# mLSTM-style attention with two MLP layers, 1 core: probabilities times v as one plain fp32 product per head

## What is computed

```
for t in range(S):                                   # the reference, a recurrence per (batch, head)
    C = f_stab * C + i_stab * outer(v_t, k_t)        # 40 x 40 state
    n = f_stab * n + i_stab * k_t
    y_t = sigmoid(o_gate_t) * (C q_t) / max(|n q_t|, 1)
x = prelu(x @ w_in, alpha) @ w_out                   # layer 1: 320 -> 2048 -> 320
out = max(x @ w1, x @ w2, x @ w3) @ w_out2           # layer 2: 320 -> 768 (three times) -> 320
```

## Time and profile before

| | us |
|---|---|
| median of 3 runs (lowest, highest) | 805.46 (802.93, 806.68) |
| span of the profiled execution, first to last instruction | 803.0 |
| PE busy in it | 754.5 (94%) |
| DVE busy | 541.9 (67%) |
| ACT busy | 298.8 (37%) |
| POOL busy | 206.7 (26%) |
| one pass of the loop (of 7) | 59.44 |

### The profile page before, as it was taken

The page is one execution under the profiler, slowest core; times in us unless marked ns, Lnnn a source line. Parts: engine busy times, 40 slices in busy tenths (PEclk is TensorE's granted clock), DMA queues, the critical chain, the costliest instruction groups (busy, mean ns, idle before and its releaser), DMA issues.

```text
span 803.0 us, 13943 instructions
## 1 busy us (share of the span) xinstructions
PE 754.5 (94%) x4658; PEld 702.0 (87%) x4658; DVE 541.9 (67%) x870; ACT 298.8 (37%) x685; POOL 206.7 (26%) x206
## 2 busy tenths in 40 slices
PE   1659999999999999999999999699999999999997
PEld 1649999999999999999999998698888888888886
DVE  7697997997997997997988985934243342434222
ACT  3535436436436436436435435331211212121211
POOL 5382432432433333333333312700000000000000
PEclk9968999999999999999999999999999999999999
DMA  6970321321311212222210009011020202000000
GB/s 197 279 236 18 119 69 41 118 67 46 113 67 62 97 67 82 77 67 89 70 67 24 0 0 283 6 39 65 1 72 1 72 0 72 0 33 1 33 1 33
DMA packets 37145, 55.93 MB, mean 70 GB/s; under 512 B 3329, under 2 KB 27458, under 8 KB 36738
## 3 DMA queue, kind: packets, MB, share of 16 engines
q1 hardware_dynamic: 36690, 54.57, 21.1%
q10 hardware_dynamic: 432, 1.06, 0.5%
HBM read 47.65 MB, written 7.96 MB: 69 GB/s over the span
## 4 chain that ended last, share of the span: by engine, by line
PE 70%; DVE 20%; issue 5%; DMA 1%; ACT 1%; SPq 1%; DVEq 0%; POOL 0%; ACTq 0%
PE bank L640 25%; PE bank L597 16%; DVE scale L936 4%; PE bank L613 4%; DVE g_lo L953 4%; PE bank L615 4%; PE bank L614 3%; PE bank L533 3%; PE bank L653 3%; PE bank L654 3%; PE bank L655 3%; DVE g_full L965 2%; PE bank L618 2%; PE bank L617 2%; DVE inner L910 2%
## 5 line engine op out<-in xcount | busy, mean ns | idle before, releaser
L597 PE MATMUL bank<-x_split,w_hi 128*128 128x384 f32 x640 | 182.9, 351 | 0.7 <-ACT x_split L738 0.7
L597 PE MATMUL bank<-x_split,w_lo 128*128 128x384 f32 x384 | 130.7, 340 | 0.0
L597 PEld LDWEIGHTS bank<-x_split,w_hi 128*128 128x128 f32 x640 | 119.1, 191 | 2.9 <-DVE g_full L965 1.8
L953 DVE TENSOR_TENSOR g_lo<-g_full,g_hi 128x384 fp32r<-128x384 f32 x128 | 104.7, 818 | 23.1 <-ACT g_hi L773 22.1
L773 ACT ACTIVATE g_hi<-g_full 128x384 fp32r<-128x384 f32 x128 | 66.6, 520 | 133.9 <-DVE g_full L965 133.9
L613 PE MATMUL bank<-g_hi,wproj 128*128 128x384 f32 x256 | 94.7, 370 | 8.9 <-DVE g_lo L953 8.1
L757 ACT ACTIVATE g_full<-bank 128x384 f32<-128x384 f32 x128 | 62.5, 488 | 99.2 <-PE bank L597 99.1
L1002 DVE TENSOR_TENSOR best<-bank,first_of_max 128x512 f32<-128x512 f32 x36 | 24.9, 692 | 108.1 <-PE bank L640 81.3
L965 DVE SCALAR_TENSOR_TENSOR g_full<-g_full,beta,bank 128x384 f32<-128x384 f32 x128 | 77.8, 608 | 17.5 <-ACT g_full L757 17.5
L615 PE MATMUL bank<-g_hi,wproj 128*128 128x384 f32 x256 | 87.0, 340 | 0.0
L614 PE MATMUL bank<-g_lo,wproj 128*128 128x384 f32 x256 | 86.7, 339 | 0.0
(11 more groups left out here) (115 smaller groups left out, 1506.1 us busy)
## 6 DMA issues: line engine op xcount, KB each, us to landing
u_bcast<-u_scratch SPq DMA_DIRECT2D x24, 512.0 KB, 4.3
kvo<-in_kvo SPq DMA_DIRECT2D x24, 484.0 KB, 3.5
out<-final SPq DMA_DIRECT2D x6, 640.0 KB, 3.4
layer_scratch<-rows SPq DMA_DIRECT2D x8, 384.0 KB, 2.4
q_t<-in_q_t SPq DMA_DIRECT2D x24, 120.0 KB
k_t<-in_k_t SPq DMA_DIRECT2D x48, 60.0 KB
wproj_raw<-in_w_out SPq DMA_DIRECT2D x1, 2560.0 KB, 16.7
w_raw<-in_w_max SPq DMA_DIRECT2D x2, 1152.0 KB, 9.7
```

Source lines behind the costliest of these rows:

```text
L597: ins = pe.matmul(ps[:, 0:T], w[:, a, f], xs[:, x, :], start=(m == 0), stop=(m == 7))
L953: dve.tensor_tensor(gl[:, j % G_SLOTS, :], gf[:, j % GF_SLOTS, :], gh[:, j % G_SLOTS, :].bitcast(F32), ALU.subtract).then_inc(g_lo_done, 1)
```

## The change

All values steps now take the form that block 0 had, with 41 columns in the place of 128, and all that served the bf16 parts is gone: the pack steps, prob_rest, prob_3, v_parts, v_rest, their semaphores and memsets, line 926 and the sum at line 910.

```diff
-DVE_LINKS = CPB * (1 + 4 + 3)
+DVE_LINKS = CPB * (1 + 3 + 3)
...
-    att = [[("gate", 0, 0)], [("gate", 0, 1), ("prepare", 1)], [("pack", 0, 0), ("pack", 0, 1)]]
+    att = [[("gate", 0, 0)], [("gate", 0, 1), ("prepare", 1)]]
...
-                [("finish", c, 1)] + more * [("pack", c + 1, 0)],
-                [("finish", c, 2)] + more * [("pack", c + 1, 1)] + later * [("prepare", c + 2)]]
+                [("finish", c, 1)],
+                [("finish", c, 2)] + later * [("prepare", c + 2)]]
...
                 if kind == "values":
-                    if isinstance(blk, int):
-                        pe.wait_ge(nat_loaded[c], 16 * (blk + 1))
-                        pe.wait_ge(prob_done, NG * ch + step[2] + 1)
-                        for k in range(HG):
-                            h = step[2] * HG + k
-                            v = VO + h * DE
-                            ins = pe.matmul(ps[:, k * COLS:(k + 1) * COLS], prob[:, h, :], nat[:, c, v:v + COLS],
-                                            start=True, stop=True)
-                    else:
...
-                            pe.matmul(ps[:, o:o + 3 * DE], high(prob[:, h, :]), v, start=(k == 0), stop=False,
...
-                            pe.matmul(ps[:, o:o + 2 * DE], high(prob_r[:, h, :]), v[:, 0:2 * DE], start=False,
...
-                            ins = pe.matmul(ps[:, o:o + DE], prob_3[:, h, :], v[:, 0:DE], start=False,
...
+                    pe.wait_ge(nat_loaded[c], 16 * (blk + 1))
+                    pe.wait_ge(prob_done, NG * ch + step[2] + 1)
+                    for k in range(HG):
+                        h = step[2] * HG + k
+                        v = VO + h * DE
+                        ins = pe.matmul(ps[:, k * COLS:k * COLS + DE], prob[:, h, :], nat[:, c, v:v + DE],
+                                        start=True, stop=True)
...
-                if kind == "pack":
...
-                        act.activation(v_parts[:, :, 0, 0:D], v, ACT.Copy).then_inc(v_hi, 1)
...
-                        act.activation(v_parts[:, :, 1, 0:D], v_r[:, :, :], ACT.Copy).then_inc(v_mid, 1)
...
-                    if not isinstance(blk, int):
-                        dve.wait_ge(prob_done, NG * ch + g + 1)
-                        dve.tensor_tensor(prob_r[:, heads, :], prob[:, heads, :], high(prob[:, heads, :]), ALU.subtract
-                                          ).then_inc(prob_rest, 1)
...
-                        dve.tensor_reduce(inner[:, heads, :],
-                                          ps[:, 0:HG * 3 * DE].rearrange("p (k n d) -> p k d n", k=HG, n=3),
-                                          mybir.AxisListType.X, ALU.add).then_inc(inner_in, 1)
+                    dve.tensor_tensor(inner[:, heads, :],
+                                      ps[:, :].rearrange("p (k d) -> p k d", k=HG)[:, :, 0:DE],
+                                      before_chunk[:, heads, :], ALU.add).then_inc(inner_in, 1)
...
-                    if not isinstance(blk, int):
-                        link(dve.tensor_tensor(inner[:, :, :], inner[:, :, :], before_chunk[:, 0:H, :], ALU.add))
...
-            pool.memset(v_parts[:, :, :, :], 0.0)
             link(pool.memset(kt[:, 1:CPB, :, :], 0.0))
-            pool.memset(v_parts[:, :, 0, D:DE], 1.0)
...
-                        pool.tensor_tensor(v_r[:, :, :], v, v_parts[:, :, 0, 0:D], ALU.subtract).then_inc(v_rest, 1)
...
-                        pool.tensor_tensor(v_parts[:, :, 2, 0:D], v_r[:, :, :], v_parts[:, :, 1, 0:D], ALU.subtract
...
-                    pool.tensor_tensor(prob_3[:, heads, :], prob_r[:, heads, :], high(prob_r[:, heads, :]), ALU.subtract
```

More of the change, by code:

```diff
@@ L108, in first_plan @@
     for s in PLAN_ATT:
-        if s[0] not in ("prepare", "pack") and not (s[0] == "finish" and s[1] + 1 < CPB):
+        if s[0] != "prepare" and not (s[0] == "finish" and s[1] + 1 < CPB):
             steps.append(s)
@@ L146, in wait @@
         eng.wait_ge(sem, value)
-def high(ap):
-    return ap.bitcast(BF16)[(slice(None),) * (len(ap.shape) - 1) + (slice(1, None, 2),)]
 def of_heads(ps):
@@ L206, in build @@
         prob, _ = sb("prob", [128, H, L], F32)
[L207 to L210, removed]
         v_w, _ = sb("v_weighted", [128, CPB, WG], F32)
@@ L289, in build @@
         decayed = sem("state_decayed")
[L291 to L296, removed]
         gated = sem("gated")
@@ L519, in attention @@
                 kind, c = step[0], step[1]
-                if kind in ("prepare", "gate", "pack", "finish"):
+                if kind in ("prepare", "gate", "finish"):
                     return
@@ L551, in attention @@
                 if kind == "values":
-                    if isinstance(blk, int):
-                        pe.wait_ge(nat_loaded[c], 16 * (blk + 1))
-                        pe.wait_ge(prob_done, NG * ch + step[2] + 1)
-                        for k in range(HG):
-                            h = step[2] * HG + k
-                            v = VO + h * DE
-                            ins = pe.matmul(ps[:, k * COLS:(k + 1) * COLS], prob[:, h, :], nat[:, c, v:v + COLS],
-                                            start=True, stop=True)
-                    else:
[L562 to L566, removed]
-                            pe.matmul(ps[:, o:o + 3 * DE], high(prob[:, h, :]), v, start=(k == 0), stop=False,
-                                      skip_group_check=True)
-                            pe.matmul(ps[:, o:o + 2 * DE], high(prob_r[:, h, :]), v[:, 0:2 * DE], start=False,
-                                      stop=False, skip_group_check=True)
-                            ins = pe.matmul(ps[:, o:o + DE], prob_3[:, h, :], v[:, 0:DE], start=False,
-                                            stop=True, skip_group_check=True)
+                    pe.wait_ge(nat_loaded[c], 16 * (blk + 1))
[5 more added lines that the diff above has]
+                                        start=True, stop=True)
                     ins.then_inc(values_out, 1)
@@ L723, in attention @@
                                    scale=-1.0).then_inc(eo_done, 1)
-                if kind == "pack":
[L726 to L729, removed]
-                        act.activation(v_parts[:, :, 0, 0:D], v, ACT.Copy).then_inc(v_hi, 1)
-                    else:
-                        act.wait_ge(v_rest, ch - CPB + 1)
-                        act.activation(v_parts[:, :, 1, 0:D], v_r[:, :, :], ACT.Copy).then_inc(v_mid, 1)
                 if kind == "turn":
@@ L875, in attention @@
                 ch = blk * CPB + c
-                if kind in ("prepare", "gate", "pack"):
+                if kind in ("prepare", "gate"):
                     return
@@ L1093, in attention @@
                         mask(c, ch)
[L1094 to L1098, removed]
-                        pool.tensor_tensor(v_r[:, :, :], v, v_parts[:, :, 0, 0:D], ALU.subtract).then_inc(v_rest, 1)
-                    else:
-                        pool.wait_ge(v_mid, ch - CPB + 1)
-                        pool.tensor_tensor(v_parts[:, :, 2, 0:D], v_r[:, :, :], v_parts[:, :, 1, 0:D], ALU.subtract
[L1103 to L1107, removed]
-                    pool.tensor_tensor(prob_3[:, heads, :], prob_r[:, heads, :], high(prob_r[:, heads, :]), ALU.subtract
-                                       ).then_inc(prob_split, 1)
                 if kind == "carry":
```

## The result

The changed kernel takes 817.75 us (median of 4 runs, 816.91 to 818.99) against 804.48 for the kernel before: ratio 1.0163, 95% interval [1.0142, 1.0184], or +13.3 us. Measured twice more, on other occasions, it gave 1.0172 [1.0155, 1.0189] and 1.0176 [1.0163, 1.0189]. The forecast was 816.3 in a range of 808 to 822, slower with a chance of 0.81. It holds, though the loss is 2.5 to 3 us larger than the 10.8 I had summed. The profiled execution took 816.91 us, its span 815.1, 12.1 more than the span before. (In each run of the changed kernel the span is 1.7 to 1.8 us shorter than the time, so the 803.0 of before stands for a time of some 804.8, near the middle of its runs and not at their lower end.)

A forecast was written before the change was run, and what follows sets the result against it. The prediction took TensorE's instruction issue to bound layer 1's loop. Dearer values steps, +13.4 us, less 2.6 us of end-of-pass waits gave +10.8 us, on a median of 805.46 us 816.3 us, range 808 to 822.

The forecast's parts named there:

- TensorE's content fills the pass: Layer 1's loop: TensorE's own instructions take 58.8 of a pass's 59.44 us, leaving some 0.6 us of standing.
- the wait at the first hidden step: Start of a pass: TensorE waits 0.09 us behind the copy-out of layer 1's result, which the change leaves alone.
- The price of a step: Loop's values step on TensorE: 0.80 us instead of 0.48, 0.32 more, 13.4 us over 42 steps.
- The doubt that the earlier trace might lie in a stretch of lower clock: The rows of the gates' transposes, 0.105 us a record, lie early, where the array may run slower.
- The rival that priced by columns: Values step: a record costs by its columns, 0.036 us for 41, a step 0.28; 794.5 us; chance 0.11.
- the one that took 0.085 us for a bare load: Values step: a load's exposed part is 0.085 us, not 0.107; a step 0.63; +3.7, 809 us; chance 0.08.
- the one that put load and stream in series: Values step: load and stream follow each other, 0.143 us a record, a step 1.03; +20.5, 826 us; chance 0.07.
- the term of -2.6 us: End of each pass: VectorE's finish starts earlier behind values and saves TensorE 7 x 0.37 = 2.6 us.
- the wait at the end of the pass: Second turn takes 0.62 us instead of 0.25, as the last project steps wait for g_lo behind VectorE's finish work.
- GpSimd's and ScalarE's lost work: Loop's splitting and packing work removed from both engines: costed at nothing, as TensorE waits for no work behind it.
- seven waits: End of the loop's passes: a TensorE wait of 0.37 us was counted in all seven.
- Start and end: Outside the loop: nothing, at best -1 us; the last layer-1 block and layer 2 hold no changed steps.

The follow-up runs named there:

- merged_slot: The kernel before with its bf16 product kept and its first pack step put into the step ahead of it: 801.88 us, ratio 0.9968.
- cols16: The changed kernel with only 16 of the 41 moving columns a head multiplied in the loop's values steps: 817.87 us, ratio 1.0162 to the kernel before.
- cols128: The changed kernel with 128 instead of 41 moving columns a head in the loop's values steps: 818.12 us, ratio 1.0167 to the kernel before.
- stat64: The changed kernel with only half of the stationary columns (64) loaded in the loop's values steps: 813.37 us, ratio 1.0114 to the kernel before.
- pe_alone: The kernel before with the fp32 values product and VectorE's short read alone, packing and splitting still done and waited for: 815.39 us, ratio 1.0132.
- late_prepare: The changed kernel with GpSimd's prepare of a block's third chunk held back until the pass's turns are done: 817.04 us, ratio 1.0151 to the kernel before.
- after_again: The changed kernel, unaltered, measured and traced again in a later set: 818.33 us, ratio 1.0172 to the kernel before.

## Why the prediction held, and where its sum was off

**The bound.** "TensorE's content fills the pass" was right, and it decided the sign: 58.8 us counted from starts, 0.6 us of wait. The pass of merged_slot, without a wait at the turn, is 59.02 us, so the count is right to 0.2 us, of which 0.09 is the wait at the first hidden step that the prediction names.

**The price of a step.** Forecast 0.80 us a step and +0.32; measured 0.81 and +0.325, 13.6 us over 42 steps. The reason held too: the load of 128 four-byte columns is the price of a record, not its moving columns (cols16, cols128) and not the record as such (stat64). The doubt that the earlier trace rows might lie in a stretch of lower clock was unfounded: the granted clock there is 1.00. The rival that priced by columns is refuted, and with it the one that took 0.085 us for a bare load and the one that put load and stream in series. By the Trainium skill ("TensorE: Matmul & The Clock Gate", loading the stationary operand) a load takes time in proportion to the stationary columns; the trace agrees, with 0.112 us for 128 and 0.058 for 64.

**The step that failed is the term of -2.6 us.** I wrote that finish starts earlier and that this buys the wait at the end of the pass. That much came: the second turn fell to 0.25 us in every pass, and pe_alone has no wait at any turn. But I costed GpSimd's and ScalarE's lost work at nothing, and asked only who waits for that work, not what GpSimd would do earlier. The mask of the third chunk moved to the end of the pass, held VectorE's g_lo for 0.9 us, and put a wait at the first turn of five passes: 5 x 0.37 = 1.9 us of the six waits of 0.38 us, 2.3 in all, that had gone. late_prepare shows that it is this mask: moved elsewhere, it leaves every turn at 0.25 us. I had also taken seven waits where there were six: the last pass of the kernel before had none (59.05 us). With the measured terms the sum is 13.6 - 2.3 + 1.9 = 13.2 us, against 13.3 to 13.8 by the medians. And the forecast of 816.3 looks better than its sum: it stood on a median of 805.46, and on the 804.48 that the four runs beside the changed kernel give, the same 10.8 us would have made 815.3. One count in the prediction was off without effect: three groups lie between scores and values, not four.

The Trainium skill ("SBUF — State Buffer", on its two separate sides) says that VectorE and GpSimd share a pair of ports, which one of them holds for a whole instruction where VectorE reads two inputs from SBUF, or where it works in a two-port mode, as by that page it does in a fp32 copy from SBUF to SBUF. The 1.48 us of g_lo, which ends with GpSimd's copy at 241.1, agree with the first, and the time of the copy of y with the second; no run here separates this lock from another cause on those two engines.

**Why the profiled spans differ by less.** They differ by 12.1 us, the medians by 13.3 or more. A pass without a wait at a turn takes 59.05 us before and 60.94 after; seven times that is 13.2, with the waits 12.8. The way to the loop gave 0.2 back, and the first pass the rest: it cost 61.30 us before and 62.70 after, 1.4 more instead of 1.9. TensorE begins it at the lower of its two clock levels, and where the clock rose differs between traces. Before, and then after:

```profile
core 0: us, PE busy (x) PEld busy (x) DVE busy (x) ACT busy (x) POOL busy (x), PEclk, DMA share, GB/s
59.24:65.67 6.43, 5.77 (x18) 5.37 (x19) 5.57 (x11) 2.43 (x7) 0.00 (x0) 0.50 0.00 0
59.00:64.35 5.35, 4.68 (x15) 4.29 (x16) 5.04 (x11) 1.34 (x4) 1.68 (x3) 0.50 0.00 0
```

At that level a matmul of 384 columns follows the one before after 0.32 us instead of 0.176, so 1.08 us less of it are worth about 0.5 us, an estimate from these rows. In after_again the lower level lasted 6.36 us, nearly as long as before, and its first pass took 63.17 us, 1.87 more than before, as a pass should by the price of six steps. So part of the small difference between the spans is chance: the three traces of the changed kernel have spans of 815.1, 816.4 and 815.4 us, and there is one trace of the kernel before.

**Start and end** behaved as said: in the first trace of the changed kernel 0.2 us less ahead of the loop (58.6 to 60.0 us in its three traces, 59.24 before), and 326.2 us behind it in all.

## What to carry to other kernels

Price a plain fp32 matmul with few moving columns by its weight loads, two a product of 0.11 us each for 128 stationary columns: three bf16 products with quick loads (0.12 us a head here) beat it (0.20 us) although they stream more columns. Where one engine bounds a loop, work taken off the others gains at most the waits for them (2.3 us here); ask what the relieved engine will then do sooner, and beside whom, and look for the wait that had kept it in step.

## What was not expected of the hardware

- A VectorE instruction beside GpSimd's work can take more than twice its time: g_lo 1.48 us instead of 0.55, a copy of 64 columns 0.61 and 0.97 instead of 0.20. Instructions that read PSUM did not show it: L914, at 240.98 beside GpSimd's copy, took its 0.60 us, and in the loop's 33 cases of L914 beside GpSimd's work the mean is 0.61, as without it.
- A weight load with 64 stationary columns between loads with 128 did not start ahead of the running matmuls: 0.25 us of idle on the load side ahead of each such group, and 0.27 us for the matmul ahead of it.
- Less work can be slower: with 6 us a pass of busy time taken from VectorE and 13 from GpSimd, the kernel before lost 0.22% [0.11, 0.33].
